# A linear-attention front end: inverting two sets of 32x32 blocks as halves of 16 with a corner product, and a second tile in another order

## What is computed

```python
k_n = k / (np.linalg.norm(k, axis=-1, keepdims=True) + 1e-06)
for t in range(S):
    y[:, :, t] = np.einsum('bhd,bhde->bhe', q[:, :, t], state)
    v_old = np.einsum('bhde,bhd->bhe', state, k_n[:, :, t])
    state = state + beta_t * np.einsum('bhd,bhe->bhde', k_n[:, :, t], v[:, :, t] - v_old)
...
h = np.maximum(x @ w_in, 0.0)
x = h * h @ w_out                     # 3072 tokens, 384 -> 2048 -> 384
...
expert = argmax(x @ w_gate); h = np.maximum(xe @ w1[e], 0.0); out = gate * (h @ w2[e])
```

## Time and profile before

| | us |
|---|---|
| median of 3 runs | 985.35 |
| lowest, highest | 981.61, 987.05 |
| the profiled execution, its own time | 980.26 |
| its span in the trace | 978.5 |
| TensorE busy in it | 898.4 (92%) |
| VectorE busy | 465.6 (48%) |
| ScalarE busy | 426.4 (44%) |
| GpSimd busy | 193.9 (20%) |

### The profile page before, as it was taken

The page is one execution under the profiler, slowest core; times in us unless marked ns, Lnnn a source line. Parts: engine busy times, 40 slices in busy tenths (PEclk is TensorE's granted clock), DMA queues, the critical chain, the costliest instruction groups (busy, mean ns, idle before and its releaser), DMA issues.

```text
span 978.5 us, 26066 instructions
## 1 busy us (share of the span) xinstructions
PE 898.4 (92%) x10408; PEld 770.5 (79%) x10409; DVE 465.6 (48%) x971; ACT 426.4 (44%) x745; POOL 193.9 (20%) x146
## 2 busy tenths in 40 slices
PE   3171999999999999999999999997999999999998
PEld 3161788788877888788888888876989898989997
DVE  6989779646744675467432124243222323223221
ACT  4051746653566347634643465651333333333332
POOL 3000000000000000000000003335686623376311
PEclk9995899999999999999999999998999999999999
DMA  7005559933764377336742795706576743362100
GB/s 317 1 11 219 196 180 313 378 135 117 273 227 133 129 250 275 132 124 225 228 142 99 226 353 205 279 1 224 174 274 225 271 161 137 129 259 74 64 20 9
DMA packets 36893, 175.85 MB, mean 180 GB/s; under 512 B 4574, under 2 KB 7812, under 8 KB 30914
## 3 DMA queue, kind: packets, MB, share of 16 engines
q1 hardware_dynamic: 30242, 144.83, 41.6%
q0 software_dynamic: 6560, 29.70, 8.6%
HBM read 147.76 MB, written 28.12 MB: 180 GB/s over the span
## 4 chain that ended last, share of the span: by engine, by line
PE 85%; DVE 9%; issue 2%; ACT 2%; DMA 1%; POOL 1%; DVEq 0%; POOLq 0%; ACTq 0%
PE HP L1112 7%; PE ACC L1125 7%; PE HP L1113 6%; PE HP L1114 6%; PE ACC L1127 6%; PE ACC L1126 6%; PE HP L1484 4%; PE ACC L1516 4%; PE ACC L1515 4%; PE ACC L1517 4%; PE HP L1486 4%; PE HP L1485 4%; PE P L1016 3%; PE P L1495 2%; PE P L1043 2%
## 5 line engine op out<-in xcount | busy, mean ns | idle before, releaser
L355 POOL TENSOR_TENSOR we_l<-raw_e,we_h 128x768 fp32r<-128x768 f32 x16 | 29.5, 1849 | 611.0 <-ACT we_h L481 611.0
L726 DVE TENSOR_TENSOR h_l<-h,h_h 128x512 fp32r<-128x512 f32 x96 | 66.4, 692 | 174.2 <-ACT h_h L455 174.1
L447 ACT ACTIVATE relu<-HP 128x512 f32<-128x512 f32 x96 | 57.4, 598 | 199.7 <-PE HP L1114 199.2
L1112 PE MATMUL HP<-x_h,ring 128*128 128x512 f32 x288 | 119.8, 416 | 0.6 <-DVE x_l L719 0.6
L1125 PE MATMUL ACC<-h_h,ring 128*128 128x512 f32 x288 | 116.9, 406 | 1.4 <-DVE h_l L726 1.4
L1113 PE MATMUL HP<-x_h,ring 128*128 128x512 f32 x288 | 113.9, 396 | 0.1
L1114 PE MATMUL HP<-x_l,ring 128*128 128x512 f32 x288 | 113.7, 395 | 0.0
L1127 PE MATMUL ACC<-h_l,ring 128*128 128x512 f32 x288 | 113.0, 392 | 0.0
L1126 PE MATMUL ACC<-h_h,ring 128*128 128x512 f32 x288 | 112.9, 392 | 0.0
L1326 POOL TENSOR_TENSOR we_l<-raw_e,we_h 128x1536 fp32r<-128x1536 f32 (+2 forms) x24 | 84.1, 3523 | 20.5 <-DMA we_h<-in_w 19.9
L1428 DVE TENSOR_TENSOR hT_l<-P,hT_h 128x512 fp32r<-128x512 f32 x60 | 38.7, 686 | 96.0 <-ACT hT_h L1377 96.0
(11 more groups left out here) (206 smaller groups left out, 1693.6 us busy)
## 6 DMA issues: line engine op xcount, KB each, us to landing
ring<-w_scratch SPq DMA_DIRECT2D x80, 768.0 KB, 4.8
raw_e<-in_w SPq DMA_DIRECT2D x16, 1536.0 KB, 6.8
w_scratch<-ring SPq DMA_DIRECT2D x16, 768.0 KB, 5.0
we_h<-in_w POOLq DMA_DIRECT2D x6, 1536.0 KB, 9.3
kT<-in_kT SPq DMA_DIRECT2D x6, 1024.0 KB, 9.0
kk<-in_k SPq DMA_DIRECT2D x6, 1024.0 KB, 8.2
qT<-in_qT SPq DMA_DIRECT2D x6, 1024.0 KB, 9.6
we_h<-in_w POOLq DMA_DIRECT2D x6, 1024.0 KB, 6.2
```

Of the source, the lines that this page charges most:

```text
L1112: pe.matmul(HP[n % 2][:, :], win_h[:, cols], x_h[:, k, :], start=k == 0, stop=False)
```

## The change

For the tiles 0 and 1, `substitute` is replaced by `substitute_halves`: both 16x16 diagonal halves of each block are inverted at once, 14 row steps, through a view of XT that has one more axis; the quarter of XT above them is cleared. XT becomes a tensor of its own. The missing 16x16 corner of each block comes from TensorE, in two products with a copy between: `left_of_corners` (Lm times the right half of Xt), `copy_left` on ScalarE into blk, `corners` (Xn times that). VectorE adds the result to the right half of Xt and turns Xt once more into Xn (`fill_blocks`). Tiles 2 to 5 are inverted as before.

Around it the hand-written order changes. On TensorE up(0, 0) is put between the corners and below_blocks(1), and up(0, 1) between below_blocks(1) and beside_blocks(1); the loop no longer issues these two. On VectorE place_X takes all four block rows for both tiles, the norms and scaling of tile 1 go ahead of the new state, row steps 1 to 6 go ahead of the right sides, and weights_lo goes ahead of rows_lo. On SyncE keys_T(2) and values(1) are issued ahead of rows(0), and queries(1), keys(2) and everything behind them wait for the corners of tile 1. No other products are put on TensorE in the time in which VectorE inverts the blocks.

```diff
--- before.py
+++ after.py
...
     Lm, MT, TT, prod, R, U, St, yT = (delta[n] for n in ("Lm", "MT", "TT", "prod", "R", "U", "St", "yT"))
-    blk, XT, Xt, Xn, C1 = delta["blocks"]
+    blk, Xt, Xn, C1 = delta["blocks"]
+    XT_wide = delta["XT"]
+    XT = XT_wide[:, 0:BLK * BLK].rearrange("p (c i) -> p c i", i=BLK)
+    XT_halves = XT_wide[:, :].rearrange("p (b x) -> p b x", b=2)[:, :, 0:HALF * BLK].rearrange("p b (c i) -> p b c i", i=BLK)
...
     LASTC = 2 * NCH - 1
+
+    def rows_before(t):
+
...
         sp.dma_start(wg[:, :, :], w_gate).then_inc(wg_in, 16)
         sp.wait_ge(zero_done, 1)
         sp.dma_start(x1_scratch[NT:NT + 1, :], zero).then_inc(x1_out, 16)
+        keys_T(2)
+        values(1)
         rows(0)
         load_x(0)
-        values(1)
+        sp.wait_ge(corner_done, 2)
+        queries(1)
         keys(2)
-        queries(1)
-        keys_T(2)
         store_pair(0)
         load_pair(NPAIR)
         for i in range(NF1 * NCH):
...
                 act.activation(blk[r, heads, :], Lm[r, heads, cols], ACT.Copy).then_inc(blk_done, 1)
 
         def place_X(t, blocks=range(C // BLK)):
...
             for g in range(2):
                 act.activation(R[:, pairs(g), :], vv[:, 8 * g:8 * (g + 1), :], ACT.Copy, scale=-1.0).then_inc(r_done, 1)
+
+        def copy_left(t, par, banks):
+            act.wait_ge(left_done, 2 * t + par + 1)
+            act.activation(blk[:, NP * par:NP * (par + 1), 0:HALF],
+                           banks[par][:, 0:NP * HALF].rearrange("p (h i) -> p h i", h=NP), ACT.Copy).then_inc(left_copied, 1)
 
         def copy_C1(t, par, banks=P):
             act.wait_ge(c1_done, 2 * t + par + 1)
@@ -529,12 +546,13 @@
         for f in range(NPAIR):
             weights_hi(f)
         for par in range(2):
+            copy_left(0, par, HP)
+        first_right_sides()
+        for par in range(2):
             copy_C1(0, par, HP)
         act.wait_ge(zeros, 4)
-        place_X(0, (0, 1))
         for par in range(2):
             copy_N(0, par, HP)
-        first_right_sides()
         diagonal_blocks(1, 0)
         for g in range(2):
...
@@ -545,11 +563,12 @@
             copy_U(1, g)
         for g in range(2):
             copy_y(0, 1, g, HP)
+        for par in range(2):
+            copy_left(1, par, early[1])
         rows_hi(0)
         act.wait_ge(x1_out, 16)
         for par in range(2):
             copy_C1(1, par)
-        place_X(1, (0, 1))
         for par in range(2):
             copy_N(1, par)
         for i in range(NF1 * NCH):
...
@@ -664,24 +684,41 @@
             dve.tensor_tensor(XT[:, :, :], XT[:, :, :], ngT[t % 2].unsqueeze(1).broadcast_to([128, BLK, BLK]),
                               ALU.mult).then_inc(xt_scaled, 1)
             dve.wait_ge(xt_scaled, 2 * t + 1)
-            dve.memset(XT[:, :, :].rearrange("p c i -> p (c i)")[:, 0:BLK * BLK:BLK + 1], 1.0).then_inc(xt_scaled, 1)
+            dve.memset(XT_wide[:, 0:BLK * BLK:BLK + 1], 1.0).then_inc(xt_scaled, 1)
+            if t < 2:
+                dve.memset(XT[:, 0:HALF, HALF:BLK], 0.0).then_inc(xt_cleared, 1)
 
         def substitute(t, lo, hi):
 
             for j in range(lo, hi):
                 n = (BLK - 1 - j) * j
                 pr = prod[:, 0:n].rearrange("p (c i) -> p c i", c=j)
-                if j == 1:
-                    dve.wait_ge(xt_scaled, 2 * t + 2)
-                after(dve, row_add, NROW * t + j - 1)
+                after(dve, row_add, rows_before(t) + j - 1)
                 dve.tensor_tensor(pr, XT[:, 0:j, j:j + 1].broadcast_to([128, j, BLK - 1 - j]),
                                   XT[:, j:j + 1, j + 1:BLK].broadcast_to([128, j, BLK - 1 - j]),
                                   ALU.mult).then_inc(row_mul, 1)
-                dve.wait_ge(row_mul, NROW * t + j)
+                dve.wait_ge(row_mul, rows_before(t) + j)
                 dve.tensor_tensor(XT[:, 0:j, j + 1:BLK], XT[:, 0:j, j + 1:BLK], pr, ALU.add).then_inc(row_add, 1)
 
+        def substitute_halves(t, lo, hi):
+
+            for j in range(lo, hi):
+                w = HALF - 1 - j
+                pr = prod[:, 0:2 * j * w].rearrange("p (b c i) -> p b c i", b=2, c=j)
+                if j == 1:
+                    dve.wait_ge(xt_scaled, 2 * t + 2)
+                after(dve, row_add, rows_before(t) + j - 1)
+                dve.tensor_tensor(pr, XT_halves[:, :, 0:j, j:j + 1].broadcast_to([128, 2, j, w]),
+                                  XT_halves[:, :, j:j + 1, j + 1:HALF].broadcast_to([128, 2, j, w]),
+                                  ALU.mult).then_inc(row_mul, 1)
+                dve.wait_ge(row_mul, rows_before(t) + j)
+                dve.tensor_tensor(XT_halves[:, :, 0:j, j + 1:HALF], XT_halves[:, :, 0:j, j + 1:HALF], pr,
+                                  ALU.add).then_inc(row_add, 1)
+
         def give_blocks(t):
-            dve.wait_ge(row_add, NROW * t + NROW)
+            dve.wait_ge(row_add, rows_before(t + 1))
+            if t < 2:
+                dve.wait_ge(xt_cleared, t + 1)
             dve.tensor_tensor(XT[:, :, :], XT[:, :, :], ngT[t % 2].unsqueeze(2).broadcast_to([128, BLK, BLK]),
                               ALU.mult).then_inc(x_scaled, 1)
             dve.wait_ge(x_scaled, t + 1)
@@ -691,6 +728,14 @@
                           XT[:, :, :].rearrange("p c i -> p i c")).then_inc(xt_out, 1)
             after(dve, n_done, 2 * t)
             dve.transpose(Xn[:, :, :].rearrange("p h c -> p c h"), XT[:, :, :]).then_inc(xn_out, 1)
+
+        def fill_blocks(t, bank):
+
+            dve.wait_ge(corner_done, t + 1)
+            dve.tensor_tensor(Xt[:, :, HALF:BLK], Xt[:, :, HALF:BLK], bank[:, :].rearrange("p (h i) -> p h i", i=HALF),
+                              ALU.add).then_inc(xt_full, 1)
+            dve.wait_ge(xt_full, t + 1)
+            dve.transpose(Xn[:, :, :], Xt[:, :, :]).then_inc(xn_full, 1)
 
         def right_sides(t, par, g):
             c = 2 * t + par
@@ -888,36 +933,38 @@
         dve.wait_ge(in_beta, 16)
         norms(0)
         scale_blocks(0)
-        substitute(0, 1, BLK - 1)
+        substitute_halves(0, 1, HALF - 1)
         give_blocks(0)
         dve.wait_ge(zeros, 4)
         for g in range(2):
             mask_scores(0, g)
         scale_values(0)
-        place_X(0, (2, 3))
+        sum_squares(1)
+        fill_blocks(0, P[0])
+        place_X(0, range(C // BLK))
         for par in range(2):
             for g in range(2):
                 rows_of_L(1, par, g, early[par][g])
-        sum_squares(1)
         diagonal_blocks(1, 1)
         turn_blocks(1)
+        norms(1)
+        scale_blocks(1)
         for g in range(2):
             new_state(0, g)
-        norms(1)
+        substitute_halves(1, 1, 7)
         for g in range(2):
             right_sides(0, 1, g)
         for g in range(2):
             mask_scores(1, g, early[0])
-        scale_blocks(1)
-        substitute(1, 1, 7)
+        substitute_halves(1, 7, HALF - 1)
+        give_blocks(1)
         for g in range(2):
             new_state(1, g)
-        substitute(1, 7, BLK - 1)
-        give_blocks(1)
-        place_X(1, (2, 3))
-        rows_lo(0)
         weights_lo(0)
         weights_lo(1)
+        rows_lo(0)
+        fill_blocks(1, ACC[0])
+        place_X(1, range(C // BLK))
         scale_values(1)
         for i in range(NF1 * NCH):
             dt, f = divmod(i, NF1)
@@ -1069,9 +1116,34 @@
             outputs_of_state(t, par)
             outputs_of_chunk(t, par)
 
+        def left_of_corners(t, banks):
+
+            pe.wait_ge(xt_out, t + 1)
+            pe.wait_ge(l_done, 4 * t + 4)
+            for par in range(2):
+                for i in range(NP):
+                    for n in range(C // BLK):
+                        r = slice(BLK * n, BLK * (n + 1))
+                        last = pe.matmul(banks[par][BLK * n:BLK * n + HALF, HALF * i:HALF * (i + 1)],
+                                         Lm[r, NP * par + i, BLK * (n % 2):BLK * (n % 2) + HALF],
+                                         Xt[r, NP * par + i, HALF:BLK], start=True, stop=True)
+                last.then_inc(left_done, 1)
+
+        def corners(t, bank):
+            pe.wait_ge(xn_out, t + 1)
+            pe.wait_ge(mt_done, 2 * t + 2)
+            for par in range(2):
+                pe.wait_ge(left_copied, 2 * t + par + 1)
+                for i in range(NP):
+                    for n in range(C // BLK):
+                        h, k = NP * par + i, slice(BLK * n, BLK * n + HALF)
+                        last = pe.matmul(bank[BLK * n:BLK * (n + 1), HALF * h:HALF * (h + 1)], Xn[k, h, :],
+                                         blk[k, h, 0:HALF], start=True, stop=True)
+            last.then_inc(corner_done, 1)
+
         def below_blocks(t, banks=P):
 
-            pe.wait_ge(xt_out, t + 1)
+            pe.wait_ge(xt_out if t >= 2 else xt_full, t + 1)
             pe.wait_ge(l_done, 4 * t + 4)
             if t == 1:
                 pe.wait_ge(s_new, 4)
...
@@ -1087,7 +1159,7 @@
 
```

(31 more changed lines are left out.)

## The result

The changed kernel takes 988.50 us in the median of 12 runs (984.15 to 991.08), the kernel before 984.28 us (now 12 runs, 981.61 to 987.79). The medians differ by 4.2 us; the ratio of the runs is 1.0038, with a 95% interval of 1.002 to 1.0056. So the change makes the kernel slower by some 4 us where 10.4 us less were forecast, and the time lies outside the range of 966 to 984. The profiled execution took 988.6 us, its span is 986.9.

What follows compares the result with a forecast made beforehand. A serial front up to 101.4 us, then TensorE, was taken to bound the kernel. Savings of 14.1 us a tile less losses gave -13.6, a clock fall +3.2: -10.4 from 985.35, about 975 us, range 966 to 984.

Steps and rivals of the forecast that it cites:

- part 2: Corner products on TensorE in both tiles: 256 records a stage at 17.6 ns, 4.5 us a stage, bounds 4.1 to 7.0.
- Rival (b): Narrow products cost 25 to 31 ns at the lower clock, 10 us back, total 982 to 985; chance 0.17.
- The shorter inversion: VectorE, first two tiles: 14 row steps instead of 30, 7.7 us instead of 21.8, saving 14.1 us a tile.
- Hidden work of VectorE and ScalarE in tile 0: Xn, masks, scaling, sum of squares and the first half's copy all hide under the narrow products; VectorE then waits.
- The solve of tile 0 at 49.4: First tile's solve on TensorE starts at 49.4 instead of 55.54, 6.1 us earlier.
- x: Dense layer's input: 10.5 us from last copy of y to first x_h, ready together with the corner, first up at 81.2.
- Given back behind the first up: First up at 81.2 to second gram's end at 102.6, net 13.6 us earlier; fall of the clock costs 3.2.
- That what the front gains passes to the end: After the serial front TensorE sets the pace in its own order, so the front's gain or loss reaches the end.
- (a): Rival: the clock does not fall behind the first up, so 13.6 us are gained, 971.8 in all; chance 0.24.
- (d): Rival: held loads delay ScalarE's cast of pair 4, past 14 us each further us delays TensorE by one; chance 0.07.
- (e): Rival: x binds the first up, only if products are quicker than 17 ns; first tile gains up to 0.4 us more.
- (c): Rival: narrow products cost 55 ns, 38 us in all, total 1013; slower from 32.6 ns a record; chance 0.06.

Runs made afterwards that it cites:

- left_wide: The changed kernel with 32 moving columns instead of 16 in the left products; no total given, first merge at 44.59 us, 0.26 later than in the changed kernel.
- stream_384: The kernel before with 384 narrow products (768 records) in TensorE's first idle time; they take 22.5 us, one run 1000.09 us beside a median of 1001.17.
- one_record: The changed kernel with bf16 operands in the four narrow stages, so each product is one record instead of two; ratio to the kernel before 0.9944.
- one_record_one_up: The changed kernel with bf16 operands in the narrow stages and only up(0, 0) moved ahead of the merges; ratio to the kernel before 0.9921.
- tile0_only: The changed kernel with halves and corner in tile 0 alone, tile 1 as in the kernel before; ratio to the kernel before 0.9991.
- filled: The changed kernel with only up(0, 0) moved and a dense 384-column product after every 16 narrow ones in three stages; ratio to the kernel before 1.0056.
- no_hold: The changed kernel without SyncE's wait for the corners of tile 1 before its later loads; ratio to the kernel before 1.0056.

## Why the prediction was wrong

**The step that failed** is part 2's price of the narrow products: "With 16 columns over four quadrants the columns are no limit at either clock, so I take 17.6 ns, 4.5 us a stage." As the time of a record it was even too high: the left products took 2.41/256 = 9.4 ns and the corner products 4.08/256 = 15.9 ns busy. But a stage is 512 instructions, two blocks of supply, and the sum has no term for supply at all: it lets a stage take as long as its records. No row shown ahead of the prediction had enough small instructions in one run to contradict that; 128 of L1084 in 3.52 us use up a block about as fast as it comes (3.46).

The trace of the kernel before did have the sign, in small:

```profile
63.67 0.73 PE L996 MATMUL P<-St,kT 48*64 48x48 f32 x36 [0.40 <-issue]
...
64.27 2.01 PE L1043 MATMUL HP<-qT,St 48*64 48x64 f32 x62
66.07 0.90 PE L1016 MATMUL P<-R,TT 64*64 64x48 f32 x25
67.32 1.36 PE L1016 MATMUL P<-R,TT 64*64 64x48 f32 x39 [0.34 <-issue]
```

With the two pairs of records that the dots stand for, these are 127 records between two gaps put down to "issue", 3.65 us from the one restart to the next. The next gap comes after 39 + 64 + 24, again 127 records, and ends at 70.94. By the counts and the period TensorE went at the pace of supply there already, which no experiment tested.

With 16 columns this cost far more. The two stages took from the first left product to the last corner product 12.6 us in tile 0 (30.98 to 43.55) and 17.3 us in tile 1 (75.89 to 93.16), where 9.0 a tile were in the sum: 3.6 and 8.3 us more. That is the first up at 93.1 instead of 81.2 (11.9).

Rival (b), narrow products at 25 to 31 ns, had the price: averaged over both tiles a record cost 29.9/1024 = 29 ns. Its total of 982 to 985 was still at least 3.5 us too low. And it was right in the price by luck, since its mechanism was another, the time in the array at the lower clock. The records' own times of 9.4 and 15.9 ns and left_wide speak against that, and stream_384 shows the true one. I took the fixed part from runs of 64 and 128 records, and a fixed price of 64 products says nothing on the 300th.

The Trainium skill has the rule, which I did not weigh: "Runtime: NRT & Kernel Launch", section "Instruction fetch mechanics", says that each engine's instruction memory is a FIFO refilled in blocks of 256 instructions (16 KiB). The packets of the page and the groups of 128 records agree with it. It also says that the cost of a boundary is mostly hidden; here it is not, 2.2 us of the 3.46 in stream_384.

**Point by point.**
- The shorter inversion: right. Its 14 row steps take from 19.98 to 27.65 us, 7.7 as worked out, the extra axis is free, clearing takes 0.27. Xt of tile 0 leads to the first left product at 30.98 (31.2).
- Hidden work of VectorE and ScalarE in tile 0: right, VectorE waited 6.4 us for the corner.
- The solve of tile 0 at 49.4: measured 53.44, 2.1 us earlier than before instead of 6.1.
- x: from the last copy of y to the first x_h was to be 10.5 us; it was 13.5 (72.02 to 85.52), because ScalarE's second copy of the left products stands ahead of it in order and came at 85.24, itself late by the gap of 4.38. Corner and x were not ready together, the corner came last.
- Given back behind the first up: forecast 21.4 + 3.2 for the clock, measured 30.5 (93.09 to 123.61). The fall of the clock came as forecast (keys 1.96, gram 1.99, solve 3.65 us) and also took in some of down(0, 0), 3.2 us where the sum has 2.1. The rest is beside_blocks(1), 5.8 us instead of 2.2, of which 2.68 is a missing block.
- That what the front gains passes to the end: about right and no more. In the two traces the second gram's end differs by 7.4 us and the span by 8.4. Over the runs the gram's end against the trace of before and the ratio go together (one_record -7.9 and -5.5 us, one_record_one_up -7.2 and -7.8, tile0_only -1.7 and -0.9, changed kernel +7.4 and +3.7), apart by up to 5 us (filled +10.3 and +5.5). Part of that may be the chip: stream_384, the kernel before on the chip of 1001 us, ends this gram at 118.62 instead of 116.19. The rest stays open.
- (a), (d) and (e) did not come up: the clock fell, the cast of pair 4 waited for nothing, and x did not bind the start. (c) has a loss only from a price of 32.6 ns; tile 0 paid 24.6 a record and tile 1 33.7 (12.6 and 17.3 us over 512), and beside_blocks(1) lost a block besides.

What stays open: how long a block takes is known only as periods (3.46 to 4.01 us where almost no transfer ran, up to 6.97 us beside the kernel's own loads), not what sets them; and how the two gaps of a stage fall depends on where in a block it starts, so a shift of a few instructions anywhere ahead could move a gap by a stage. This was not tried.

## What to carry to other kernels

Count instructions, not only their time: in these runs a stage of several hundred TensorE instructions whose records take less than about 27 ns for load and matmul together (an estimate, 3.46 us / 128) went at the pace of supply, and slower beside heavy loads. Such a stage is made shorter by fewer records, not by smaller products; 16-bit operands did it here where the precision allows, larger tiles were not tried. Halving work on one engine by handing it as many tiny products to another can cost all that it saves, so look for the packets of the instruction queue and for gaps at equal counts in the trace.

## What was not expected of the hardware

- Groups of exactly 128 records with 2.2 us between them while TensorE had nothing to wait for (stream_384). An idle stretch of 14 us ahead of a stage brings no more: 157 records (314 instructions) went at the first start in the changed kernel, and then it stopped.
- Narrow records are very short: 9.4 ns for 32x16 on 16 columns, 14.7 ns with 32 columns (2.31/157), 15.9 for 16x32 on 16. In stream_384, at 9.8 ns, the granted clock was 0.50.
- Transfers of the kernel's own data slow the arrival of TensorE's instructions: one period of 6.97 us in no_hold against 3.68 in the changed kernel, at the same products.
